# Attention and two feed-forward layers on one core: the second layer by seven products instead of eight

## What is computed

```python
attn = softmax(window_mask(scale * q @ k.T)) @ v     # 4 x 8 heads, 576 keys, window 64
x = attn as (2304, 512)
h = maximum(maximum(x @ w1, x @ w2), x @ w3)         # layer 1: 512 -> 768
y = h @ w_out                                        # layer 2: 768 -> 512
s = y @ moe2_w_in                                    # layer 3: 512 -> 2048
g = where(s >= 1, s, where(s <= -1, 0, (s + 1)**2 / 4))
out = g @ moe2_w_out                                 # layer 4: 2048 -> 512
```

## Time and profile before

| | before |
|---|---|
| median of 3 runs (lowest to highest) | 745.77 us (745.68 to 748.2) |
| the profiled execution | 745.96 us |
| its span | 744.1 us |
| layer 2 by the chain of waits | from 291.67 us, 74.90 us, 432 matmuls |
| layer 3 begins | 366.58 us |
| VectorE, ScalarE, GpSimd busy in layer 2 | 28.4, 31.8, 34.2 us |

### The profile page before, as it was taken

One profiled execution on the slowest core, in us unless ns is written; L12 is line 12 of the kernel. 1 busy time (PEld: TensorE's weight loads), 2 busy tenths in 40 slices (PEclk: granted clock), 3 DMA queues, 4 the chain that ended last, 5 costly groups with the idle time before them and its releaser, 6 DMA issues.

```text
span 744.1 us, 12661 instructions
## 1 busy us (share of the span) xinstructions
PE 736.4 (99%) x4706; PEld 653.0 (88%) x4706; DVE 302.1 (41%) x746; ACT 330.0 (44%) x795; POOL 309.6 (42%) x237
## 2 busy tenths in 40 slices
PE   8999999999999999999999999999999999999998
PEld 6998888888888888999998989989899898999986
DVE  4642242143222024353047532644644453266334
ACT  6854443444520201454255543474554455245332
POOL 4631221111110520566068752676774376267321
PEclk9999999999999999999999999999999999999999
DMA  9842321221002100110011020011220004001302
GB/s 338 301 147 89 102 89 59 61 88 31 28 0 85 57 1 0 57 56 0 0 57 58 0 85 1 1 72 42 76 67 2 1 0 145 25 2 57 114 0 86
DMA packets 24040, 46.18 MB, mean 62 GB/s; under 512 B 2224, under 2 KB 3632, under 8 KB 23984
## 3 DMA queue, kind: packets, MB, share of 16 engines
q1 hardware_dynamic: 23552, 44.93, 17.8%
q10 hardware_dynamic: 432, 0.49, 0.2%
HBM read 37.55 MB, written 7.86 MB: 61 GB/s over the span
## 4 chain that ended last, share of the span: by engine, by line
PE 96%; DMA 1%; ACT 1%; DVE 1%; issue 0%; SPq 0%; DVEq 0%
PE wide L566 29%; PE wide L647 26%; PE bank L627 24%; PE wide L600 10%; PE bank L538 2%; PE wide L514 2%; PE bank L523 2%; DMA q<-q_dram 1%; PE wide L551 1%; ACT prob L669 1%; DVE part_in L994 0%; ACT pT L684 0%; ACT h L694 0%; ACT safe L678 0%; PE wide L573 0%
## 5 line engine op out<-in xcount | busy, mean ns | idle before, releaser
L566 PE MATMUL wide<-xT,w 128*128 128x512 f32 (+1 forms) x1032 | 228.4, 377 | 0.0
L566 PEld LDWEIGHTS wide<-xT,w 128*128 128x128 f32 x1032 | 180.5, 188 | 34.4 <-issue 1.7
L647 PE MATMUL wide<-w4s,gT 128*128 128x512 f32 x864 | 205.6, 391 | 0.0
L647 PEld LDWEIGHTS wide<-w4s,gT 128*128 128x128 f32 x864 | 161.3, 188 | 32.1 <-POOL gT L1045 0.5
L1045 POOL TENSOR_TENSOR gT<-g,gT 128x384 fp32r<-128x384 f32 x96 | 111.3, 1169 | 175.5 <-ACT gT L664 175.5
L627 PE MATMUL bank<-yT,w3s 128*128 128x384 f32 x1008 | 183.6, 336 | 0.0
L627 PEld LDWEIGHTS bank<-yT,w3s 128*128 128x128 f32 x1008 | 177.2, 188 | 4.1 <-DVE g L986 0.3
L968 DVE TENSOR_TENSOR pu<-bank,pu 128x384 f32<-128x384 f32 x72 | 40.1, 557 | 174.9 <-PE bank L627 173.0
L1053 POOL TENSOR_TENSOR prob<-prob,row_inv 128x512 f32<-128x512 f32 x36 | 38.1, 1062 | 153.4 <-DVE row_inv L884 153.3
L791 ACT ACTIVATE g_sq<-g_sq,half 128x384 f32<-128x384 f32 x96 | 58.9, 616 | 85.4 <-DVE g_sq L980 83.4
L898 DVE TENSOR_TENSOR h<-wide,h 128x512 f32<-128x512 f32 (+1 forms) x60 | 38.1, 635 | 94.1 <-PE wide L566 93.9
(11 more groups left out here) (56 smaller groups left out, 539.5 us busy)
## 6 DMA issues: line engine op xcount, KB each, us to landing
v<-v_dram SPq DMA_DIRECT2D x36, 256.0 KB, 4.1
raw<-w_dram SPq DMA_DIRECT2D x16, 512.0 KB, 3.6
h<-moe_w_dram SPq DMA_DIRECT2D x12, 384.0 KB, 6.7
k<-k_dram SPq DMA_DIRECT2D x16, 288.0 KB, 4.3
q<-q_dram SPq DMA_DIRECT2D x16, 256.0 KB, 4.0
part_dram<-o_sb SPq DMA_DIRECT2D x12, 256.0 KB, 2.0
part_in<-part_dram SPq DMA_DIRECT2D x2, 1536.0 KB, 7.0
out_dram<-part_in SPq DMA_DIRECT2D x11, 256.0 KB, 2.1
```

What stands on the lines that cost most here:

```text
L566: mm = pe.matmul(acc[bank][:, cols], w123[:, wp, w, kc, c * P:(c + 1) * P], xT[:, x_side(t), xp, kc, 0:TOKENS[t]], start=(kc == x == 0), s ...
L647: mm = pe.matmul(acc4[b], gT[:, k, gp, tb * P:(tb + 1) * P], w4s[pair_f(g) % HALF_F][:, wp, f, :], start=(first and x == 0), stop=(last an ...
```

## The change

Layer 2 is computed on three pairs of token tiles (`TILE_PAIRS`) by the same scheme that layer 3 has: the input's halves (channels 0 to 383 and 384 to 767, `KH` = 3 chunks) by the two tiles of a pair, and the weight's four quarters, are combined into seven operands each. The seven products m of a pair t run in order, each for two output chunks j, with 3 x 3 = 9 matmuls each: 3 x 7 x 2 x 9 = 378. The seven input operands `h_ops[m]` have one buffer each. Four are sums or differences (`sum_of_h`, VectorE), all seven get a high part (`h_high`, ScalarE) and a low part (`h_low`: m = 0 to 5 of pair 0 and 0 to 4 of pairs 1 and 2 by VectorE, the rest by GpSimd), each of 128x1152. The results are collected in `h1` by copies (`l2_copy`, `l2_last`, ScalarE) and additions out of PSUM (`l2_add`, VectorE), for which TensorE waits. GpSimd prepares the weight in seven casts, seven low parts and four sums of 128x768 during layer 1's last tile. The first three sums of pair 0 and the low parts m = 0 and 1 of it are put into VectorE's order of layer 1's last tile. `load_w3(0)` waits for low parts 3 and 5 of pair 0, since the sums lie where the raw weights come. The low parts of `yT` for m = 2 and 5 of the first version go from GpSimd to VectorE (`y_low`). The first product of layer 3 waits for the addition before the last one.

The diff, cut to its core: semaphores, part of the placement and small guards are left out, and so are the lines taken away, which are L590 to L603, `h1_parts`, `y_chunk` and L761 to L781 of ScalarE, `h1_low` and L949 to L960 of VectorE, and L1078 to L1085 and L1111 to L1117 of GpSimd in the code above:

```diff
+    if engine == "DVE":
+        at = LAYER1_AT[-1]
+        later += [(at + 8.2, "h_low", 0), (at + 9.2, "h_low", 1), (at + 13.2, "h_sum", 0), (at + 14.2, "h_sum", 1),
+                  (at + 15.2, "h_sum", 2)]
...
+    wo1, at = place("wo1", [P, 2, PRODUCTS, KH, 2 * P], F32R, A_AT)
+    h_ops = [None] * PRODUCTS
+    for m in range(2):
+        h_ops[m], at = place(f"h_op{m}", [P, 2, KH, MTOK], F32R, at)
+    for m in range(2, PRODUCTS):
+        h_ops[m], _ = place(f"h_op{m}", [P, 2, KH, MTOK], F32R, A_AT - 4 * 2 * KH * MTOK * (PRODUCTS - m))
+    wo1_sums, end = place("wo1_sums", [P, 2, KH, 2 * P], F32, X_AT + 4 * 2 * KC * MOST)
...
+            late_sums, _ = place("late_sums", [P, 2, KH, MTOK], F32, at - W4_BYTES)
+            t_sums, at = place("t_sums", [P, 3, 2, MTOK], F32, at)
             yT, at = place("yT", [P, PRODUCTS, 2, 2, MTOK], F32R, at)
...
+    def l2_banks(t, j):
+        two = p_ps if j == 0 else acc4
+        return two[(t + 1) % 2], two[t % 2]
...
+    def h_operand(t, m):
+        return {0: h_half(t, 0, 0), 1: h_half(t, 1, 0), 2: h_sums(t)[:, 1, :, :], 3: h_sums(t)[:, 0, :, :],
+                4: h_half(t, 0, 1), 5: h_sums(t)[:, 1, :, :], 6: h_half(t, 1, 1)}[m]
...
+        sp.wait_ge(h_lo[3], 1)
+        sp.wait_ge(h_lo[5], 1)
...
+        def layer2(t, m, j):
+            a, c = l2_banks(t, j)
+            if j == 0:
+                pe.wait_ge(h_lo[m], t + 1)
+            if t == m == j == 0:
+                pe.wait_ge(wo1_lo, PRODUCTS)
+            if m == 0:
+                after(pe, l2_added, 6 * (t - 1) + 4 + j + 1)
+            elif m == 1:
+                after(pe, l2_out, 2 * (t - 1) + j + 1)
+            elif m == 2:
+                pe.wait_ge(l2_copied, 6 * t + j + 1)
+            elif m == 3:
+                pe.wait_ge(l2_added, 6 * t + j + 1)
+            elif m == 4:
+                pe.wait_ge(l2_copied, 6 * t + 2 + j + 1)
+            elif m == 5:
+                pe.wait_ge(l2_copied, 6 * t + 4 + j + 1)
+            else:
+                pe.wait_ge(l2_added, 6 * t + 2 + j + 1)
+            bank = c if m in (1, 3, 5) else a
+            for kc in range(KH):
+                for x, (wp, hp) in enumerate(PASSES):
+                    mm = pe.matmul(bank[:, 0:MTOK], wo1[:, wp, W_OF[m], kc, j * P:(j + 1) * P], h_ops[m][:, hp, kc, :],
+                                   start=(m in (0, 1, 3) and kc == x == 0), stop=(kc == KH - 1 and x == 2),
+                                   skip_group_check=True)
+            mm.then_inc(l2_made, 1)
+        for t in range(TILE_PAIRS):
+            for m in range(PRODUCTS):
+                for j in range(2):
+                    layer2(t, m, j)
...
+                if g == 0:
+                    pe.wait_ge(l2_added, 6 * TILE_PAIRS - 1)
...
+        def h_high(t, m):
+            if t > 0:
+                act.wait_ge(l2_made, 2 * PRODUCTS * (t - 1) + 2 * (m + 1))
+            if m in (2, 3, 4, 5):
+                act.wait_ge(h_sum, 4 * t + (3, 1, 2, 4)[m - 2])
+            hi(h_ops[m][:, 0, :, :], h_operand(t, m)).then_inc(h_hi[m], 1)
+        def l2_copy(t, n):
+            if n == 0:
+                act.wait_ge(h_sum, 4 * t + 2)
+            elif n == 1:
+                act.wait_ge(h_sum, 4 * t + 4)
+            else:
+                act.wait_ge(h_lo[4], t + 1)
+                act.wait_ge(h_lo[6], t + 1)
+            for j in range(2):
+                act.wait_ge(l2_made, 2 * PRODUCTS * t + 2 * (0, 2, 3)[n] + j + 1)
+                act.activation(y_chunk(t, j, (0, 2, 1)[n]), l2_banks(t, j)[(0, 0, 1)[n]][:, 0:MTOK], ACT.Copy).then_inc(l2_copied, 1)
+        def l2_last(t):
+            for j in range(2):
+                act.wait_ge(l2_made, 2 * PRODUCTS * (t + 1) - 1 + j)
+                act.activation(y_chunk(t, j, 3), l2_banks(t, j)[0][:, 0:MTOK], ACT.Copy).then_inc(l2_out, 1)
...
+                act.wait_ge(l2_made, 2 * PRODUCTS * (TILE_PAIRS - 1) + 2 * ((2, 3, 4, 4, 5, 6, 6)[m] + 1))
...
+        h_high(0, 0)
+        h_high(0, 1)
         for b in range(2):
             act.wait_ge(acc_free[b], GROUPS // 2 * L1_TILES + ACC_CREDIT)
+        for m in (2, 3, 4, 6):
+            h_high(0, m)
+        l2_copy(0, 0)
+        h_high(0, 5)
+        for t in range(TILE_PAIRS):
+            more = t + 1 < TILE_PAIRS
+            if more:
+                h_high(t + 1, 0)
+                h_high(t + 1, 1)
+            l2_copy(t, 1)
+            if t > 0:
+                w4_parts(t - 1)
+            if not more:
+                act.wait_ge(l2_added, 6)
+                y_part(0, 0)
+            l2_copy(t, 2)
+            if more:
+                h_high(t + 1, 2)
+                h_high(t + 1, 3)
+                w3_parts(t, 0)
+                w3_parts(t, 1)
+                h_high(t + 1, 4)
+            else:
+                for m in range(1, 5):
+                    y_part(0, m)
+            l2_last(t)
+            if more:
+                h_high(t + 1, 6)
+                l2_copy(t + 1, 0)
+                h_high(t + 1, 5)
+                w3_parts(t, 2)
+        y_part(0, 5)
+        y_part(0, 6)
+        act.wait_ge(l2_added, 6 * TILE_PAIRS)
...
+        def h_low(t, m):
+            dve.wait_ge(h_hi[m], t + 1)
+            lo(h_ops[m][:, 1, :, :], h_operand(t, m), h_ops[m][:, 0, :, :]).then_inc(h_lo[m], 1)
+        def sum_of_h(t, n):
+            b11, b12, b21, b22 = (h_half(t, k, tile) for k in range(2) for tile in range(2))
+            t3, t2 = (h_sums(t)[:, i, :, :] for i in range(2))
+            if n == 0:
+                if t == 0:
+                    dve.wait_ge(wo1_lo, PRODUCTS)
+                elif t == 1:
+                    for b in range(2):
+                        dve.wait_ge(acc_free[b], GROUPS // 2 * L1_TILES + ACC_CREDIT)
+                else:
+                    dve.wait_ge(h_lo[3], t)
+                dve.tensor_tensor(t3, b22, b12, ALU.subtract).then_inc(h_sum, 1)
+            elif n == 1:
+                dve.wait_ge(h_sum, 4 * t + 1)
+                dve.tensor_tensor(b12, b12, b11, ALU.subtract).then_inc(h_sum, 1)
+            elif n == 2:
+                dve.wait_ge(h_sum, 4 * t + 2)
+                if t == 2:
+                    dve.wait_ge(h_lo[5], t)
+                dve.tensor_tensor(t2, b22, b12, ALU.subtract).then_inc(h_sum, 1)
+            else:
+                dve.wait_ge(h_lo[2], t + 1)
+                dve.tensor_tensor(t2, b21, t2, ALU.subtract).then_inc(h_sum, 1)
+        def l2_add(t, n):
+            for j in range(2):
+                dve.wait_ge(l2_made, 2 * PRODUCTS * t + 2 * (1, 4, 5)[n] + j + 1)
+                dve.wait_ge(l2_copied, 6 * t + 2 * (0, 2, 1)[n] + j + 1)
+                to = y_chunk(t, j, n)
+                dve.tensor_tensor(to, l2_banks(t, j)[(1, 0, 1)[n]][:, 0:MTOK], to, ALU.add).then_inc(l2_added, 1)
...
+        def y_low(m):
+            dve.wait_ge(t_hi, m + 1)
+            lo(yT[:, m, 1, :, :], t_sums[:, 1, :, :], yT[:, m, 0, :, :]).then_inc(t_lo[m], 1)
+        h_low(0, 2)
+        sum_of_h(0, 3)
+        h_low(0, 3)
+        l2_add(0, 0)
+        h_low(0, 4)
+        h_low(0, 5)
+        for t in range(1, TILE_PAIRS):
+            for n in range(3):
+                sum_of_h(t, n)
+            h_low(t, 0)
+            l2_add(t - 1, 1)
+            h_low(t, 1)
+            l2_add(t - 1, 2)
+            h_low(t, 2)
+            sum_of_h(t, 3)
+            h_low(t, 3)
+            weight_sums(t - 1)
+            l2_add(t, 0)
+            h_low(t, 4)
+        dve.wait_ge(l2_out, 2)
+        dve.wait_ge(l2_added, 6)
         for n in range(3):
             y_sum(0, n)
+        l2_add(TILE_PAIRS - 1, 1)
+        weight_sums(2)
+        y_low(2)
         y_sum(0, 3)
+        l2_add(TILE_PAIRS - 1, 2)
+        y_low(5)
...
+        a11, a12, a21, a22 = (src[:, KH * k:KH * (k + 1), c * 2 * P:(c + 1) * 2 * P] for c in range(2) for k in range(2))
+        def wo1_parts(n, operand, source):
+            pool.tensor_copy(wo1[:, 0, operand, :, :], source).then_inc(wo1_hi, 1)
+            pool.wait_ge(wo1_hi, n + 1)
+            lo(wo1[:, 1, operand, :, :], source, wo1[:, 0, operand, :, :]).then_inc(wo1_lo, 1)
+        wo1_parts(0, A11, a11)
+        wo1_parts(1, A12, a12)
+        wo1_parts(2, A22, a22)
+        s3, s1 = (wo1_sums[:, i, :, :] for i in range(2))
+        pool.tensor_tensor(s3, a11, a21, ALU.subtract).then_inc(wo1_sum, 1)
+        pool.tensor_tensor(s1, a21, a22, ALU.add).then_inc(wo1_sum, 1)
+        pool.wait_ge(wo1_sum, 1)
+        wo1_parts(3, S3, s3)
+        pool.wait_ge(wo1_sum, 2)
+        wo1_parts(4, S1, s1)
+        pool.wait_ge(wo1_lo, 5)
+        pool.tensor_tensor(s1, s1, a11, ALU.subtract).then_inc(wo1_sum, 1)
+        pool.wait_ge(wo1_sum, 3)
+        wo1_parts(5, S2, s1)
+        pool.wait_ge(wo1_lo, 6)
+        pool.tensor_tensor(s1, a12, s1, ALU.subtract).then_inc(wo1_sum, 1)
+        pool.wait_ge(wo1_sum, 4)
+        wo1_parts(6, S4, s1)
...
+        h_low(0, 6)
         for j in range(2):
+            w3_part(j, 0)
```

(58 more changed lines are left out.)

73 lines of the change are left out of this document (30 added, 43 removed).

## The result

| | before | after |
|---|---|---|
| median (lowest to highest) | 745.71 us (745.48 to 748.21, 8 runs) | 749.59 us (747.92 to 750.54, 8 runs) |
| after / before | | 1.0048, 95% interval 1.0039 to 1.0058 |
| profiled execution, its span | 745.96, 744.1 | 747.92, 746.1 |
| VectorE, GpSimd busy in the span | 302.1, 309.6 us | 357.0, 338.5 us |

The change makes the kernel slower, by 3.9 us between the medians, although TensorE has 54 matmuls less. (The measured ratio is 1.0048; the quotient of the two medians is 1.0052.) The profiled execution of after is the quickest of its eight, 2.0 us over that of before.

What follows compares the result with a forecast made beforehand. TensorE, 99% busy, bounds the kernel before; VectorE and GpSimd sharing a port would then delay it. From 745.96: -9.36 matmuls, +13.4 stalls, +1.9 clock gives 751.9, median 751.7 us, range 739 to 757.

Steps and rivals of the forecast that it cites:

- the case: Main forecast: port turns delay layer 2 and layer 3's start; 751.7 us, own range 748 to 757, chance 0.60 with (d).
- slower: Outcome of the whole kernel over 749.5 us; chance 0.58.
- same: Outcome of the whole kernel between faster (under 742.0 us) and slower (over 749.5); chance 0.22.
- The turns at the port: Layer 2: VectorE's two-SBUF-input instructions and GpSimd's exclude each other; 71.2 us of common queue against 63.5 available.
- rival (a): Layer 2: the port doesn't bind, low parts find gaps; 737.3 us, chance 0.14.
- the walk: Instruction-by-instruction layout of layer 2 into layer 3 with engine order, semaphores and port turns; 13.4 us of stalls.
- The weight: Layer 1's last tile: GpSimd prepares layer 2's weight by 274.3, VectorE asks at 278.8; slack 4.5 us, no cost.
- Rival (c): Layer 1's last tile: GpSimd's weight late by over 4.5 us, so TensorE stands; 755 us and up, chance 0.08.
- The stalls: TensorE waits for VectorE's additions in pairs 1 and 2 and before layer 3: 0.9, 2.7, 2.2, 7.5; 13.4 us.
- The clock: Layer 3's start: the idle lowers TensorE's granted clock, costing 1.9 us, bounds 0 and 7.3.
- rival (d): Layer 3's start: change as told but the idle doesn't lower the clock; 749.8 us, chance within the forecast's 0.60.
- Rival (b): Before layer 3: port binds, but weight_sums(2) and y_low(2) precede y_part; 743 us (740.5 to 747), chance 0.18.

Runs made afterwards that it cites:

- e1_memset: The changed kernel with GpSimd's low parts from after w_out's preparation to layer 3's first period written as zeros, without reading SBUF: 736.85 us, ratio 0.9881 to before.
- e5_memset3: As e1_memset, but each zero fill done three times, so that GpSimd works as long as in the changed kernel: 737.38 us, ratio 0.9888 to before.
- e4_keep_busy: The changed kernel with 44 more unused matmuls on TensorE between layer 2's end and its wait for layer 3: 747.48 us, ratio 1.0022 to before.
- e7_splits_first: The changed kernel with additions l2_add(t - 1, 1) and (t - 1, 2) behind low parts h_low(t, 1) and (t, 2): 748.80 us, ratio 1.0034 to before.
- e2_sums_later: The changed kernel with weight_sums(2) moved from ahead of y_low(2) to the end of layer 3's first period: 743.99 us, ratio 0.9981 to before.
- e9_order_y_first: e6_order with GpSimd's w4_part(1) moved behind the low parts 0, 1, 3 and 4 of y: 741.08 us, ratio 0.9937 to before.
- e10_order_halves: e6_order with GpSimd's low parts there each done as two instructions of half the columns: 743.54 us, ratio 0.9963 to before.
- e6_order: The changed kernel with only VectorE's order changed: three l2_add additions earlier, weight_sums(2) at the end of layer 3's first period: 740.59 us, ratio 0.9933 to before.

## Why the prediction was right, and where it was off

Forecast 751.7 us, measured 749.59, inside the range of 739 to 757 and inside the case's own of 748 to 757. Of the three chances, "slower" (0.58) and "same" (0.22) can't be told apart: 749.59 is just over the 749.5 where "slower" began, the ratio of 1.0048 just under 0.5%, and its interval of 1.0039 to 1.0058 holds the bound. That the number came out so near is in part luck: the stalls were forecast 3.0 us too long, and the medians differ by 1.9 us more than the two profiled executions; that of after, which the sum below explains, took 747.92, just under the case's own range.

- **The matmuls.** 378 at 0.173, 9.36 us less: right.
- **The turns at the port** were the step on which the case hung, and e1_memset and e5_memset3 show it. Without GpSimd's reads the time is 736.85 and 737.38, where rival (a) had 737.3: the turns, with the clock's fall behind them, cost 12 to 13 us. VectorE's 128x1152 instruction alone takes 1.35 us (1.36 in the walk).
- **The weight.** GpSimd's first cast and last low part of it in after:

```profile
242.31 0.83 POOL L1252 CAST wo<-stage 128x768 fp32r<-128x768 f32 x1 [32.66 <-PE wide L610]
268.09 2.84 POOL L1215 TENSOR_TENSOR wo<-wo_sums,wo 128x768 fp32r<-128x768 f32 x1
```

  A cast is 0.83 us instead of 1.00, and the weight is ready at 270.9 instead of 274.3. Rival (c) didn't occur; TensorE goes into layer 2 at 290.98 without a wait.
- **The stalls.** 10.4 us instead of 13.4: layer 2 from 291.16 to 360.98 is 69.8 us for 65.5 of matmuls, so 4.3 inside it, and 6.15 behind. By places, forecast to measured: product 3 of pair 1 0.9 to under 0.1, product 6 of pair 1 2.7 to 2.2, product 3 of pair 2 2.2 to 1.75, layer 3's start 7.5 to 6.15. The term that was mis-sized is the overlap at a turn, where I let the next instruction start 0.08 us before the end of the last. From one pair of turns to the next there are 359.09 - 357.11 = 1.98 us where the walk has 0.42 + 1.85 - 0.16 = 2.11, and 328.60 - 326.23 = 2.37 where it has 2.48. That is 0.1 us for each pair of turns. From the end of `weight_sums(0)` to the end of the addition that layer 3 waits for, the walk has 370.4 - 323.0 = 47.4 us, after 367.02 - 321.63 = 45.4: 2.0 less. The other 0.9 had come by then (321.63 instead of 323.0, of which 0.5 is layer 2's earlier start); of what, I didn't settle.
- **The clock.** 1.9 forecast from the earlier trace rows; 9.87 - 8.32 = 1.55 in the profile; 2.1 in medians by e4_keep_busy. The size was right, and rival (d) falls.
- **The sum** in the profiled executions: -9.36 + 4.3 + 6.15 + 1.55 = +2.6; from the start of layer 2 to the first piece of layer 4, before 291.67 to 374.90, after 291.16 to 376.99, the difference is 85.83 - 83.23 = 2.6. After's layer 1 ended 0.5 us sooner, which leaves the 2.0 of the two profiled executions. The medians differ by 3.9. The remaining 1.9 isn't in the profile of after, its quickest execution. Its cause stays open, but the profile of e7_splits_first, whose execution took 749.58 us, shows where such an amount can lie: the same 36 matmuls in layer 1 begin at 101.83 instead of 100.27, long before anything that the change or the edit touches, and the 48 matmuls behind the wait take 10.75 instead of 9.87.
- **Rival (b)** named what e2_sums_later then did by edit: the last part packed better. It had 743 (740.5 to 747); 743.99 was measured.

## What to carry to other kernels

Count the elementwise work that a change adds by the resource that it shares, here VectorE's two-input instructions and GpSimd's together, and not engine by engine: 48% and 45% of the span looks like room, and in layer 2 VectorE was at work or blocked 68.2 of 70 us. Where two engines take turns, a short instruction pays the full length of the other's, so keep short ones (four weight sums) away from the place just before something that TensorE waits for: moving them brought 5.6 us, and the whole order 9.0, without less work. Before a seven-product scheme is judged, the order of its engines has to be tried: here the same work in another order went from 0.48% slower than the plain product to 0.67% faster.

## What the runs showed of the hardware beyond what I expected

- The clock's fall has no fixed price: the same 48 matmuls behind a wait of 5.2 to 6.7 us took 9.87, 10.13, 10.27 and 10.75 us in four kernels' profiles, and 8.56 with TensorE kept at work.
- The clock fell behind short waits too: one of 2.03 us in e9_order_y_first, two of 1.33 in e10_order_halves. In e6_order, with five waits of 0.2 to 0.85, it stayed at 1.00.
- GpSimd's zero fill takes 1.06 us for 128x1152, its difference of two tensors 2.77 where VectorE held it up least in after (at 317.79), and the fills leave VectorE alone even at 43.6 us in all in layer 2.
- VectorE's waits at the port follow the length of GpSimd's single instruction: 2.9 us for a weight sum beside 128x1152, 2.06 beside 128x768, 1.65 beside 128x576.
